# Picking the first expert's tokens on TensorE by products with tables of slots, in place of reading them back from DRAM

## The reference

```python
# attention, B=4, H=8, S=576, D=64; heads 0..3 look at the last 32 positions, 4..7 at every 32nd
scores = np.where(masks, scale * q @ k.T, -1e9)
attn = softmax(scores) ; x = (attn @ v) laid out as (2304 tokens, 512)

# mixture of experts, E=8, 512 -> 1024 -> 512, for tokens with x @ w_skip > 0
e_idx = argmax(x @ w_gate) ; gate_w = softmax(x @ w_gate)[e_idx]
for e in range(8):
    h = relu(x[e_idx == e] @ w1[e])
    y[e_idx == e] = gate_w * (h @ w2[e])
x = x + y

# dense block, 512 -> 2048 -> 512
h = x @ w_in
g = where(h >= 1, h, where(h <= -1, 0, (h + 1)**2 / 4))
out = g @ w_out
```

## Time and profile before

| | |
|---|---|
| runs | 687.99, 693.4, 691.78 us; median 691.78 |
| the profiled execution | 691.78 us; its span, first to last instruction, 690.0 us |
| PE busy | 648.0 us, 94% of the span |
| DVE busy | 314.8 us, 46% |
| ACT busy | 187.9 us, 27% |
| POOL busy | 126.9 us, 18% |
| mean granted TensorE clock | 0.974 |

### The profile page before, as it was taken

The page is one execution under the profiler, slowest core; times in us unless marked ns, Lnnn a source line. Parts: engine busy times, 40 slices in busy tenths (PEclk is TensorE's granted clock), DMA queues, the critical chain, the costliest instruction groups (busy, mean ns, idle before and its releaser), DMA issues.

```text
span 690.0 us, 12493 instructions
## 1 busy us (share of the span) xinstructions
PE 648.0 (94%) x5190; PEld 553.9 (80%) x5195; DVE 314.8 (46%) x570; ACT 187.9 (27%) x361; POOL 126.9 (18%) x135
## 2 busy tenths in 40 slices
PE   7888856899999999899999999999999999999995
PEld 3767642899999999788888888888888888888994
DVE  4766250141122121675446644456545565545652
ACT  2545450141111111222224222233222332223331
POOL 1323145002222224882000200002000020000201
PEclk9999986999999999999999999999999999999998
DMA  8676495964777775330000100001000010000100
GB/s 285 225 257 226 166 359 198 352 228 167 262 253 255 257 258 178 94 106 16 1 0 1 62 0 1 0 1 61 0 0 0 0 61 0 0 0 0 62 1 30
DMA packets 39477, 76.34 MB, mean 111 GB/s; under 512 B 3079, under 2 KB 17844, under 8 KB 38916
## 3 DMA queue, kind: packets, MB, share of 16 engines
q1 hardware_dynamic: 36556, 66.26, 28.1%
q0 software_dynamic: 2880, 9.52, 3.6%
HBM read 65.83 MB, written 9.94 MB: 110 GB/s over the span
## 4 chain that ended last, share of the span: by engine, by line
PE 81%; DMA 9%; POOL 3%; DVE 2%; issue 1%; SPq 1%; ACT 1%; DVEq 0%
PE pair L1043 28%; PE pair L1056 16%; PE bank L1056 13%; PE pair L1000 9%; DMA WE<-w 4%; PE out_pair L1010 4%; PE bank L1010 4%; DMA k_str<-kT 2%; POOL x_sorted L456 2%; PE out_pair L895 2%; PE pair L853 2%; DMA k_loc<-kT 1%; PE bank L873 1%; DMA xfirst<-x_sorted 1%; PE out_pair L937 1%
## 5 line engine op out<-in xcount | busy, mean ns | idle before, releaser
L1043 PE MATMUL pair<-yh,WIH 128*128 128x512 f32 (+1 forms) x320 | 116.7, 371 | 0.2 <-ACT yh L596 0.2
L1043 PE MATMUL pair<-yh,WIL 128*128 128x512 f32 (+1 forms) x320 | 116.5, 370 | 0.0
L620 ACT ACTIVATE cl<-cl,half 128x512 f32<-128x512 f32 (+1 forms) x80 | 54.5, 681 | 186.9 <-DVE cl L808 185.5
L816 DVE TENSOR_TENSOR gl<-gr,gh 128x512 fp32r<-128x512 f32 (+1 forms) x80 | 54.1, 677 | 73.6 <-ACT gh L629 72.5
L808 DVE TENSOR_SCALAR cl<-pair 128x512 f32<-128x512 f32 (+1 forms) x80 | 50.9, 637 | 73.0 <-PE pair L1043 73.0
L515 POOL DMA_INDIRECT out<-XT,tok x18 | 18.6, 1031 | 351.6 <-DVE XT L796 347.6
L1043 PE MATMUL pair<-yl,WIH 128*128 128x512 f32 (+1 forms) x320 | 79.7, 369 | 1.7 <-DVE yl L787 1.7
L1000 PE MATMUL pair<-xw,WE 128*128 128x168 f32 x512 | 76.2, 311 | 0.2
L1000 PEld LDWEIGHTS pair<-xw,WE 128*128 128x128 f32 x512 | 74.8, 193 | 0.8 <-DMA WE<-w 0.7
L1043 PEld LDWEIGHTS pair<-yh,WIH 128*128 128x128 f32 x320 | 60.7, 190 | 11.3 <-ACT yh L596 0.6
L629 ACT CAST gh<-gr 128x512 fp32r<-128x512 f32 (+1 forms) x80 | 46.3, 579 | 86.0 <-PE bank L1056 61.0
(11 more groups left out here) (144 smaller groups left out, 814.4 us busy)
## 6 DMA issues: line engine op xcount, KB each, us to landing
WE<-w SPq DMA_DIRECT2D x16, 2048.0 KB, 12.3
xrow<-x_sorted SPq DMA_DIRECT2D x6, 781.5 KB, 9.1
v_loc<-vl SPq DMA_DIRECT2D x4, 1024.0 KB, 7.8
raw_in<-win SPq DMA_DIRECT2D x16, 256.0 KB, 9.5
raw_out<-wout SPq DMA_DIRECT2D x16, 256.0 KB, 2.6
q_loc<-qT SPq DMA_DIRECT2D x4, 576.0 KB, 6.1
k_loc<-kT SPq DMA_DIRECT2D x4, 576.0 KB, 8.1
v_str<-vs SPq DMA_DIRECT2D x8, 256.0 KB, 4.2
```

The source lines that it names most:

```text
L620: act.activation(cl[:, 0:n], cl[:, 0:n], ACT.Square, bias=half[:, :], scale=0.5).then_inc(squared, 1)
L816: dve.tensor_tensor(gl[:, f % 2, 0:n], gr[:, 0:n], gh[:, f % 2, 0:n].bitcast(F32), ALU.subtract).then_inc(g_low, 1)
L1043: last = pe.matmul(h2_b[f % 2][:, 0:tokens], w[:, c, P * f:P * (f + 1)], x[:, c, 0:tokens], start=(k == 0), stop=(k == 3 * DC - 1))
```

## The change

Expert 0's window is no longer read back from DRAM. For each row tile DVE makes a table `hot(t)`, 128 tokens by 168 slots, which is 1 where the token's slot is that column, and 0 elsewhere (one comparison of a row of numbers 0 to 167, `slots`, with `posf`). PE multiplies each block of 128 features of the row tile by the table and sums over the 18 tiles: 72 products, which give the turned window of expert 0 directly. The tables lie in `XT`, whose tokens have by then been turned into `xrow`. The 40 products on the mask go. Expert 1's window is still read back, into `xsecond`; its 8 transposes now stand behind into(0). SP's six loads of the sorted rows now also wait for the end of the 72 products, which read `xrow`.

```diff
-C_COLS = C_I + 1
+C_SLOT = C_I + 1
+C_COLS = C_SLOT + WIN
...
-        first_b, sort_b = bank[2:6], bank[2:6]
+        first_b, second_b, sort_b = bank[4:8], bank[2:4], bank[2:6]
...
+        def hot(t):
+
+            return XT[:, t % DC, WIN * (t // DC):WIN * (t // DC + 1)]
...
@@ SP
-                    sp.dma_start(pairs[:, :], cst[0:EXTRA, C_END:C_COLS]).then_inc(pairs_in, 16)
+                    sp.dma_start(slots[:, :], cst[:, C_SLOT:C_COLS]).then_inc(slots_in, 16)
+                    sp.dma_start(pairs[:, :], cst[0:EXTRA, C_END:C_SLOT]).then_inc(pairs_in, 16)
...
-            sp.wait_ge(scattered, 16 * BUSY_FROM)
-            for signal in late_out:
-                sp.wait_ge(signal, 16)
-            for par in range(2):
-                sp.dma_start(xfirst[:, 2 * par, :], xs[bass.ds(start_1 if par else 0, P), 0:D]).then_inc(first_in[par], 16)
-                sp.dma_start(xfirst[0:WIN - P, 2 * par + 1, :], xs[bass.ds(start_1 + P if par else P, WIN - P), 0:D]).then_inc(first_in[par], 16)
-
+            sp.wait_ge(scattered, 16 * NT)
+            sp.dma_start(xsecond[:, 0, :], xs[bass.ds(start_1, P), 0:D]).then_inc(second_in, 16)
+            sp.dma_start(xsecond[0:WIN - P, 1, :], xs[bass.ds(start_1 + P, WIN - P), 0:D]).then_inc(second_in, 16)
+
+            sp.wait_ge(first_picked, 1)
             for g in range(NS):
...
@@ ACT
             act.wait_ge(more_ready, 1)
-            for par in range(2):
-                act.wait_ge(first_turned, 2 * par + 2)
-                act.copy(xw[:, par, :, P:WIN], first_b[2 * par + 1][:, 0:DC * (WIN - P)].rearrange("p (c n) -> p c n", c=DC)).then_inc(first_rest, 1)
+            act.wait_ge(first_picked, 1)
+            for c in range(1, DC, 2):
+                act.copy(xw[:, 0, c, :], first_b[c][:, 0:WIN]).then_inc(first_copied, 1)
...
             relus(0, 0)
+            act.wait_ge(second_turned, 2)
+            act.copy(xw[:, 1, :, P:WIN], second_b[1][:, 0:DC * (WIN - P)].rearrange("p (c n) -> p c n", c=DC)).then_inc(second_copied, 1)
...
@@ DVE
             dve.tensor_copy(slot_of[:, :], posf[:, :]).then_inc(slots_ready, 1)
+            dve.wait_ge(slots_in, 16)
+            for t in range(NT):
+                dve.tensor_scalar(hot(t), slots[:, :], posf[:, t:t + 1], None, ALU.is_equal).then_inc(hot_ready, 1)
             link(dve.tensor_copy(starts[:, :], base[0:1, :, 0]))
...
-            for par in range(2):
-                dve.wait_ge(first_turned, 2 * par + 1)
-                dve.tensor_copy(xw[:, par, :, 0:P], first_b[2 * par][:, :].rearrange("p (c n) -> p c n", c=DC)).then_inc(first_main, 1)
+            dve.wait_ge(first_picked, 1)
+            for c in range(0, DC, 2):
+                dve.tensor_copy(xw[:, 0, c, :], first_b[c][:, 0:WIN]).then_inc(first_copied, 1)
+            dve.wait_ge(second_turned, 1)
+            dve.tensor_copy(xw[:, 1, :, 0:P], second_b[0][:, :].rearrange("p (c n) -> p c n", c=DC)).then_inc(second_copied, 1)
...
@@ PE
             pe.wait_ge(rows_copied, NT)
             pe.wait_ge(slots_ready, 1)
-            for t in range(BUSY_FROM, NT):
-                pe.wait_ge(late_out[t - BUSY_FROM], 16)
-                for _ in range(BUSY_SCATTER + (BUSY_LOAD if t == NT - 1 else 0)):
-                    pe.matmul(bank[0][:, :], ident_b[:, :], mask_b[:, 0, :].unsqueeze(1).to_broadcast([P, 8, KEYS]), start=True, stop=True)
-            for par in range(2):
-                pe.wait_ge(first_in[par], 32)
+
+            for t in range(NT):
+                pe.wait_ge(hot_ready, t + 1)
+                for c in range(DC):
+                    last = pe.matmul(first_b[c][:, 0:WIN], xrow[:, t, P * c:P * (c + 1)], hot(t), start=(t == 0), stop=(t == NT - 1))
+            last.then_inc(first_picked, 1)
+
+            def second_rows():
+                pe.wait_ge(second_in, 32)
...
-                pe.wait_ge(first_main, 2)
-                pe.wait_ge(first_rest, 2)
+                pe.wait_ge(second_copied, 2)
...
             into(0, 0, 0, 1)
+            second_rows()
             sort_turned()
             into(1, 1, 1, 1)
```

More of the change, by code:

```diff
@@ L80 @@
 BUSY_VALUED = [4, 0, 2, 2]
-BUSY_FROM, BUSY_SCATTER, BUSY_LOAD = 10, 4, 8
 SLOTS = TB
@@ L161, in program @@
         raw_out, _, raw_end = at("raw_out", [P, 2, D], F32)
-        xfirst, _, o = at("xfirst", [P, 4, D], F32, i_at)
+        xsecond, _, o = at("xsecond", [P, 2, D], F32, i_at)
         assert o <= raw_end
@@ L187, in program @@
         n_more, _, _ = at("n_more", [1, 1], I32)
-        pairs, _, _ = at("pairs", [EXTRA, C_COLS - C_END], F32)
+        pairs, _, _ = at("pairs", [EXTRA, C_SLOT - C_END], F32)
         slot_of, _, _ = at("slot_of", [P, NT], U32)
@@ L215, in program @@
         value, _, o = at("value", [EXTRA, 2], F32, o)
+        slots, _, o = at("slots", [P, WIN], F32, o)
         assert o <= h_end
@@ L251, in program @@
         scattered, pads_out = sem("scattered"), sem("pads_out")
-        late_out = [sem(f"late_out{t}") for t in range(BUSY_FROM, NT)]
-        first_in = [sem(f"first_in{i}") for i in range(2)]
-        first_turned, first_main, first_rest = sem("first_turned"), sem("first_main"), sem("first_rest")
+        slots_in, hot_ready, first_picked, first_copied = sem("slots_in"), sem("hot_ready"), sem("first_picked"), sem("first_copied")
+        second_in, second_turned, second_copied = sem("second_in"), sem("second_turned"), sem("second_copied")
         sorted_in = [sem(f"sorted_in{g}") for g in range(NS)]
@@ L393, in start_of @@
                 return sp.value_load(starts[0:1, bass.ds(e, 1)], min_val=0, max_val=N)
-            sp.wait_ge(first_turned, 4)
+            sp.wait_ge(second_turned, 2)
             for par in range(2):
@@ L455, in _ @@
                 pool.wait_ge(rows_copied, t + 1)
-                pool.indirect_dma_start(xs, bass.IndirectOffsetOnAxis(slot_of[:, t:t + 1], 0), xrow[:, t, :], None).then_inc(scattered if t < BUSY_FROM else late_out[t - BUSY_FROM], 16)
+                pool.indirect_dma_start(xs, bass.IndirectOffsetOnAxis(slot_of[:, t:t + 1], 0), xrow[:, t, :], None).then_inc(scattered, 16)
             def start_of(e):
@@ L961, in _ @@
             pe.wait_ge(slots_ready, 1)
-            for t in range(BUSY_FROM, NT):
-                pe.wait_ge(late_out[t - BUSY_FROM], 16)
-                for _ in range(BUSY_SCATTER + (BUSY_LOAD if t == NT - 1 else 0)):
-                    pe.matmul(bank[0][:, :], ident_b[:, :], mask_b[:, 0, :].unsqueeze(1).to_broadcast([P, 8, KEYS]), start=True, stop=True)
-            for par in range(2):
-                pe.wait_ge(first_in[par], 32)
+            for t in range(NT):
[5 more added lines that the diff above has]
+                pe.wait_ge(second_in, 32)
                 for r, rows_ in ((0, P), (1, WIN - P)):
                     for c in range(DC):
-                        last = pe.transpose(first_b[2 * par + r][:, rows_ * c:rows_ * (c + 1)], xfirst[0:rows_, 2 * par + r, P * c:P * (c + 1)], ident[0:rows_, 0:rows_])
-                    last.then_inc(first_turned, 1)
+                        last = pe.transpose(second_b[r][:, rows_ * c:rows_ * (c + 1)], xsecond[0:rows_, r, P * c:P * (c + 1)], ident[0:rows_, 0:rows_])
+                    last.then_inc(second_turned, 1)
             def sort_turned():
-                pe.wait_ge(first_main, 2)
-                pe.wait_ge(first_rest, 2)
+                pe.wait_ge(second_copied, 2)
                 for t in range(NT):
@@ L991, in into @@
                 pe.wait_ge(w1_in[par], 16 * loads)
-                if isinstance(e, int) and e < 2:
-                    pe.wait_ge(first_main, e + 1)
-                    pe.wait_ge(first_rest, e + 1)
+                if isinstance(e, int) and e == 0:
+                    pe.wait_ge(first_copied, DC)
+                elif isinstance(e, int) and e == 1:
+                    pe.wait_ge(second_copied, 2)
                 else:
@@ L1105, in host_constants @@
     c[0:EXTRA, C_I] = np.arange(1, EXTRA + 1)
+    c[:, C_SLOT:C_COLS] = np.arange(WIN)[None, :]
     return c
```

## The result

| | before | after |
|---|---|---|
| median of 4 runs each, side by side | 689.88 us (687.21 to 693.4) | 682.01 us (680.93 to 682.94) |
| the profiled execution | 691.78 us, span 690.0 | 681.35 us, span 679.4 |
| mean granted TensorE clock | 0.974 | 0.994 |

The ratio, from runs taken side by side, is 0.9883, with a 95% interval of 0.9851 to 0.9916: the medians put the changed kernel 7.9 us, or 1.2%, ahead, and the interval allows 5.8 to 10.3 us. The forecast was 685.0 us and "within 1%" as the likelier side. The time lies at the lower edge of the range, and the kernel is measurably faster.

A forecast was written before the change was run, and what follows sets the result against it. PE is busy from 146.2 us, so moving into(1) moves the end; before it PE waits on row copies, scatters and loads. 7.8 gained, less 0.4 (scatters) and 0.6 (`slots`), is 6.8: 691.8 to 685.0 us, range 682 to 689.3.

The forecast's parts named there:

- the main term: Last row copy to sort_turned: 40 products and both waits gone, into(0) at full clock, transposes and bubble inserted; 7.8 us gained.
- S: Time at which sort_turned starts on PE: 136.3 us before, forecast 128.5 us; the work behind it is unchanged.
- The pause of 1.2 us ahead of the picks: PE's pause after 96.4 us of work; forecast to leave the full clock for picks and into(0).
- the scatters' term: DVE's tables beside POOL's scatters: scatters delayed 1.5 us, 1.1 of it hidden, 0.4 us lost, range 0 to 2.2.
- the term of `slots`: One more load in batch 1 delays the queries and keys PE waits for; 0.6 us lost, bounds 0 and 0.9.
- rival 2: Clean case: scatters not disturbed and the load of `slots` hidden; gain 7.8 us, 684.0 us; chance 0.13.
- Rival 1: Tables block POOL's scatters fully, which land 3.3 us later; gain 5.0 us, 686.8 us; chance 0.2.
- rival 4: POOL's scatters hold up DVE's tables, into(0) starts 2.7 us later; gain 4.5 us, 687.3 us; chance 0.07.
- Rival 3: PE's clock falls behind the pause ahead of the picks, losing 1.7 or 2.6 us; gain 4.6, 687.2 us; chance 0.1.
- Rival 5: Picks at half clock throughout, too loose from waits on tables, take 41 us; kernel 705.5 us; chance 0.03.
- The margin of 1.1 us: In sort_turned: last sorted rows land 0.6 to 1.5 us before PE needs them, 1.1 in the middle.
- The products on the mask: 40 products on PE before into(0), 11.50 us; said to buy a full clock for the next stage, which picks now give.

The follow-up runs named there:

- The long copies: Changed kernel with eight extra DVE copies inside `XT`, behind the list of surplus windows and beside POOL's scatters; 683.89 us in one run.
- the load alone: Kernel before with only the load of `slots` and DVE's wait for it added; 689.11 us, ratio 1.0012.
- the one trace with a pause of 2.79 us: Profiled execution, 687.72 us, of the changed kernel with one wait for all 18 tables ahead of the picks; that kernel's median 681.41 us, ratio 0.9851.
- the second set: Changed kernel again, without an edit, 695.85 us, ratio 1.0099; beside it early picks, half of the picks, and early picks with into(1) ahead of sort_turned.
- the fourth set's control: Changed kernel run again without an edit, against the kernel before; 682.21 us, ratio 0.9897.
- picks 1.4 us earlier: Changed kernel with each tile's picks waiting for that tile's row copy alone instead of all 18; 683.73 us, ratio 0.9927.

## Why the prediction came out as it did

**Right: what bounds the kernel, and the price of the main term.** The 7.8 us that the prediction worked out at S were 7.9 in the pair of traces. Its parts also hold: 20.5 us of picks forecast and 20.48 measured (0.285 us a product), into(0) 21.5 and 21.6 us behind the last row copy, into(0) in 9.1 and 9.2 us, 1.5 and 1.4 us of transposes and bubble behind it. The pause of 1.2 us ahead of the picks was there, and left the clock at 1.00.

**Wrong: the scatters' term.** The step "Tables are short, with gaps, so I take a delay near the middle, 1.5 us", of which 0.4 were to be lost, measured 0.13 us (21.81 us from first to last scatter, 21.68 before), with nothing lost. A table took 0.23 us, just under the forecast 0.25 to 0.34, and begun one cast behind `slot_of` the row of them overlapped three scatters. The prediction split the difference between free and fully blocked. The long copies show where between them it lies: at most part of one instruction, 0.38 us, for a scatter that meets one, and nothing for another.

**Wrong, as far as it can be told: the term of `slots`.** For the step "Since PE was waiting, nothing covers it", with 0.6 us lost, no cost is seen: the wait for the keys is 1.2 us in the changed kernel and 1.4 with the load alone, not 3.3. The 2.70 us of the earlier trace rows were one trace's, and what the wait is there differs by more than an issue's time from run to run: 1.2 and 2.1 us in two traces of the changed kernel. The 10 runs with the load alone cannot tell 0.6 us from nothing, so this step is unsupported rather than disproved.

**The side.** These two terms, 1.0 us of cost against 7.8 of gain, moved the likeliest case from just over 1% to just under it, and so put 0.56 on "within 1%". Either term alone would have left it over 1% (7.8 less 0.4 or 0.6 of 691.8), so the side hung on the two small costs together. With both at zero the forecast is rival 2's, which had 0.13: 7.8 us, and 7.9 were measured. The other 1.9 us between 685.0 and 682.01 lie in the base: three runs before gave 691.78, more of them 689.2 to 690.4.

**The rivals.** Rival 1 (blocked scatters) and rival 4 (tables held up by the scatters) did not occur: the 18 tables stand 0.233 us apart beside the scatters. Rival 3 (clock) did not occur behind the pause of 1.16 us, and did in the one trace with a pause of 2.79 us. Rival 5 put the break-even at 0.38 us a product. Picks did run at 0.45 to 0.5 us a product in the second set, and the kernel was slower, but not for rival 5's reason, half clock from loose waits: there were gaps in issue with the operands ready, and the clock fell only behind the first of them. Nothing in the trace before pointed to that.

**The sorted rows.** The margin of 1.1 us was the right place to look. It holds in the first trace of the changed kernel (no wait, where 0.4 us was forecast), is used up by 0.5 us in the fourth set's control, is gone with picks 1.4 us earlier, and takes all of the 10 us that half of the picks would give.

**The products on the mask** were misjudged ("what they bought, a full clock for the next stage"), without effect on the sum.

## What to carry to other kernels

Work put into a stretch in which a slow transfer sets the end is worth what it takes off the path behind, up to the next thing that is late; price that first, since here halving the picks gained nothing at into(1). Where a cost is bounded by "none" and "fully", and neither end was seen, taking the middle of several such terms biases the sum: here both were near zero. Such a change is to be measured on more than one chip: the same program was 1.0 to 1.2% faster in three sets of runs and 1.0% slower in a fourth.

## What the runs showed of the hardware

- A dense row of float32 products beside a row of indirect scatters can lose its issue for up to 1.9 us at a time, on one chip and not on others, while the kernel before was the same on all. On that chip the count raised by the last product came 9.7 us behind its end in one trace, 0.01 us in the same kernel's trace on another chip. The cause is open.
- A POOL scatter that meets DVE copies inside SBUF waits for part of one (1.34 us in place of 0.96 beside copies of 0.6 us) or for none, so that 4.0 us of copies cost the row of scatters 0.4 us.
- A stretch of nothing but transposes, sort_turned, kept a granted clock of 1.00 for 9.8 us. With half of the picks it began at 0.50 and reached 1.00 before any other product ran.
- 40 products on a mask ahead of a wait of 2.3 us bought nothing: ratio 1.0006 without them.
